# Splitting the gate weights earlier, and dividing the row sums one slot ahead, in a fused attention and mixture kernel

## The reference

```python
scores = scale * np.matmul(q, k.transpose(0, 1, 3, 2))
kth = np.partition(scores, -32, axis=-1)[..., -32:-31]
scores = np.where(scores >= kth, scores, -1e9)
attn = np.exp(scores - np.max(scores, axis=-1, keepdims=True))
attn = attn / (np.sum(attn, axis=-1, keepdims=True) + 1e-09)
x = (attn @ v), heads side by side           # 1152 x 512

rms = np.sqrt(np.mean(x * x, axis=-1, keepdims=True) + 1e-06)
xn = x / rms * rms_g
g = xn @ w_gate                              # 512 x 1536
x = (g * sigmoid(g) * (xn @ w_val)) @ w_out

expert_idx = np.argmax(x @ r_gate, axis=1)   # 8 experts, 288 places each
out[i] = gate_w[i] * relu(x[i] @ w1[e]) @ w2[e]
```

## Time and profile before

| | before |
|---|---|
| median of 3 runs | 669.05 us (667.72 to 669.4) |
| profiled execution | 668.76 us |
| its span | 667.0 us |
| PE busy | 615.8 us, 92% |
| DVE busy | 418.3 us, 63% |
| ACT busy | 326.3 us, 49% |
| POOL busy | 258.7 us, 39% |
| mean granted clock of PE | 0.984 of 2.4 GHz |
| chain that ended last | PE 76%, ACT 8%, POOL 6%, issue 4%, SP's queue 3% |

### The profile page before, as it was taken

The page is one execution under the profiler, slowest core; times in us unless marked ns, Lnnn a source line. Parts: engine busy times, 40 slices in busy tenths (PEclk is TensorE's granted clock), DMA queues, the critical chain, the costliest instruction groups (busy, mean ns, idle before and its releaser), DMA issues.

```text
span 667.0 us, 11082 instructions
## 1 busy us (share of the span) xinstructions
PE 615.8 (92%) x3914; PEld 475.3 (71%) x3914; DVE 418.3 (63%) x915; ACT 326.3 (49%) x713; POOL 258.7 (39%) x361
## 2 busy tenths in 40 slices
PE   5767879999999999999999999999989999999994
PEld 3445655775774775775765766756669999999994
DVE  4999899799699798898897997921111110111110
ACT  3485874765865766756756766742211011111110
POOL 1285874444544555464364463552310101111101
PEclk9997999999999999999999999999979999999998
DMA  9999200010010000000000000000395677667501
GB/s 187 339 373 371 59 18 1 1 33 0 1 33 2 12 22 1 18 17 0 17 17 2 1 17 0 1 17 0 130 391 186 216 230 276 223 223 283 167 1 37
DMA packets 53070, 65.45 MB, mean 98 GB/s; under 512 B 32218, under 2 KB 32218, under 8 KB 53020
## 3 DMA queue, kind: packets, MB, share of 16 engines
q1 hardware_dynamic: 51276, 60.05, 27.7%
q0 software_dynamic: 1744, 4.76, 2.0%
HBM read 52.89 MB, written 12.30 MB: 98 GB/s over the span
## 4 chain that ended last, share of the span: by engine, by line
PE 76%; ACT 8%; POOL 6%; issue 4%; SPq 3%; DMA 2%; DVE 1%; POOLq 0%; ACTq 0%
PE ps L746 11%; PE ps L760 11%; PE ps L514 11%; PE ps L501 8%; PE ps L505 7%; PE ps L502 7%; PE ps L482 5%; PE ps L455 4%; PE ps L466 4%; POOL s_ring L1409 3%; PE ps L440 3%; ACT pt L819 2%; DMA w_loads<-in_moe_w_gate 2%; POOL hid L1352 2%; ACT z_pair L957 1%
## 5 line engine op out<-in xcount | busy, mean ns | idle before, releaser
L1409 POOL TENSOR_TENSOR s_ring<-s_ring,z_pair 128x576 f32<-128x576 f32 x72 | 100.9, 1422 | 68.9 <-ACT z_pair L957 68.9
L1232 DVE MATCH_REPLACE8 w_top<-m,w_top 128x576 f32<-128x576 f32 x144 | 105.8, 742 | 0.0
L1228 DVE MAX8 m<-w_top 128x8 f32<-128x576 f32 x144 | 101.6, 746 | 0.0
L514 PE MATMUL ps<-wo_space,hid 128*128 128x512 f32 x216 | 99.3, 593 | 0.4 <-issue 0.4
L501 PE MATMUL ps<-w_parts,x_hi 128*128 128x512 f32 x216 | 90.2, 418 | 1.8 <-DVE w_parts L1161 1.1
L502 PE MATMUL ps<-w_parts,x_hi 128*128 128x512 f32 x216 | 85.4, 395 | 0.0
L746 PE MATMUL ps<-arena,w_loads 128*128 128x168 f32 x512 | 76.6, 312 | 0.6 <-ACT arena L819 0.6
L760 PE MATMUL ps<-arena,w_loads 128*128 128x168 f32 x512 | 75.9, 307 | 0.5 <-issue 0.5
L746 PEld LDWEIGHTS ps<-arena,w_loads 128*128 128x128 f32 x512 | 75.5, 195 | 1.0 <-ACT arena L819 1.0
L760 PEld LDWEIGHTS ps<-arena,w_loads 128*128 128x128 f32 x512 | 73.2, 190 | 0.6 <-issue 0.6
L1430 POOL DMA_INDIRECT out_rows<-arena,s_ring x16 | 15.1, 942 | 150.7 <-DVE arena L1256 113.6
(11 more groups left out here) (133 smaller groups left out, 875.3 us busy)
## 6 DMA issues: line engine op xcount, KB each, us to landing
w_loads<-in_moe_w SPq DMA_DIRECT2D x16, 2048.0 KB, 9.0
dispatched_rows<-drow SPq DMA_DIRECT2D x18, 260.0 KB, 7.2
w_loads<-in_moe_w_gate SPq DMA_DIRECT2D x1, 3072.0 KB, 11.7
w_loads<-in_moe_w_val SPq DMA_DIRECT2D x1, 3072.0 KB, 19.9
wo_space<-in_moe_w_out SPq DMA_DIRECT2D x1, 3072.0 KB, 14.1
arena<-dispatched_rows SPq DMA_DIRECT2D x8, 341.2 KB
out_rows<-drow SPq DMA_DIRECT2D x9, 256.0 KB, 5.3
q_space<-in_q SPq DMA_DIRECT2D x8, 256.0 KB, 3.0
```

The lines of the kernel that those rows point to most:

```text
L514: last = mm(blk[0], hid[:, c * P:(c + 1) * P], wo_s[:, c, :], start=(c == 0), stop=(c == CF - 1))
L1228: vec.max(m8[:, 2 * (n % 2) + a, i, :], w_top[:, a, :]).then_inc(s["top_step"], 1)
L1232: vec.match_replace(w_top[:, a, :], m8[:, 2 * (n % 2) + a, i, :], w_top[:, a, :], NEG).then_inc(s["top_step"], 1)
L1409: gp.tensor_tensor(row, row, z_pair[:, a, :], ALU.subtract).then_inc(s["lowered"], 1)
```

## The change

- SP issues `w_gate` right behind the first keys, and the keys of batch 1 ahead of the values of batch 0.
- The pieces are numbered anew: 0 to 5 are the gate's, 6 to 11 the value's. ACT writes their high parts in slots 0 to 3, 5 and 6 (two each, GAMMA); POOL writes all twelve low parts, in slots 1 to 7; `LOW_VECTOR` is gone. A block of tile 0 waits for the pieces that it needs, counted in the order of `LOW`.
- `divide(t, part)` takes the sum and the power out of `norm_first`. Part 0 (6 heads) runs on POOL at the end of slot 4t+3, in every tile, behind `dense(n, GAMMA)`; part 1 (2 heads) runs in slot 4t+4 behind the scaling.
- In group 3 alone ACT takes the second exponential ahead of the next scores' copies.
- For tile 0 alone, `low_part` runs on DVE inside the search of group 5, between its first replace pair and the next MAX8, instead of behind that search.
- For tile 0 alone, PE runs 2 extra matmuls (`bridge`) in slot 5.

```diff
-EARLY = (8, 3, 4, 3)
+EARLY = (8, 3, 4, 3, 2)
-HIGH = ((1, GAMMA), (1, GAMMA), (2, GAMMA), (2, GAMMA), (4, GAMMA), (5, BETA),
-        (5, GAMMA), (5, GAMMA), (6, ALPHA), (6, GAMMA), (6, GAMMA), (7, ALPHA))
-LOW = {0: (2, ALPHA), 1: (2, ALPHA), 2: (3, ALPHA), 3: (3, ALPHA), 4: (5, BETA), 5: (5, BETA), 6: (6, ALPHA), 7: (6, BETA), 11: (7, BETA)}
-LOW_VECTOR = {8: (6, GAMMA), 9: (7, ALPHA), 10: (7, ALPHA)}
+HIGH = ((0, GAMMA), (0, GAMMA), (1, GAMMA), (1, GAMMA), (2, GAMMA), (2, GAMMA),
+        (3, GAMMA), (3, GAMMA), (5, GAMMA), (5, GAMMA), (6, GAMMA), (6, GAMMA))
+LOW = {0: (1, ALPHA), 1: (1, ALPHA), 2: (2, ALPHA), 3: (2, ALPHA), 4: (3, ALPHA), 6: (4, ALPHA), 7: (5, ALPHA),
+       8: (6, ALPHA), 9: (6, BETA), 5: (6, GAMMA), 10: (7, ALPHA), 11: (7, BETA)}
+LOW_ORDER = tuple(LOW)
...
+            sp.dma_start(wg_raw, w_gate.rearrange("(c p) f -> p c f", p=P)).then_inc(s["wg_in"], 16)
+            key_rows(1, s["k_in1"])
             value_rows(0, s["v_in0"])
             q_tile(1, 0)
-            key_rows(1, s["k_in1"])
             sp.dma_start(gain[:], rms_g.rearrange("(c p) -> p c", p=P), allow_slow_non_contiguous=True).then_inc(s["g_in"], 16)
-            sp.dma_start(wg_raw, w_gate.rearrange("(c p) f -> p c f", p=P)).then_inc(s["wg_in"], 16)
             sp.dma_start(wv_raw, w_val.rearrange("(c p) f -> p c f", p=P)).then_inc(s["wv_in"], 16)
...
-                    pe.wait_ge(s["w_lo_set"], sum(p < m for p in LOW))
+                    pe.wait_ge(s["w_lo_set"], low_ready(i, bank is blk[1]))
...
+                if t == 0:
+                    pe.wait_ge(s["k1_copied"], KC)
+                    bridge(EARLY[4])
                 pe.wait_ge(s["normed"], 2 * t + 2)
...
                     if here:
                         probs(g, 0)
+                        if g == HP - 1:
+                            probs(g, 1)
...
-            def low_part(n):
+            def low_part(n, first=False):
                 t = due(n, ALPHA, XB)
-                if t is not None:
+                if t is not None and first == (t == 0):
...
                     if a == 0:
                         beside(n - 1, GAMMA)
+                low_part(n, True)
...
-            def norm_first(t):
-
-                pool.wait_ge(s["masked"], (t + 1) * H)
+            def divide(t, part):
+
+                h0, h1 = ((0, H - 2), (H - 2, H))[part]
+                pool.wait_ge(s["masked"], t * H + h1)
                 if t > 0:
                     pool.wait_ge(s["normed"], 2 * t)
-                gp.tensor_scalar(rden[:], den[:, t % 2, :], EPS_SUM, None, ALU.add).then_inc(s["den_step"], 1)
-                pool.wait_ge(s["den_step"], 2 * t + 1)
-                gp.tensor_tensor(rden[:], rden[:], nones[:], ALU.pow).then_inc(s["den_step"], 1)
-                pool.wait_ge(s["den_step"], 2 * t + 2)
+                gp.tensor_scalar(rden[:, h0:h1], den[:, t % 2, h0:h1], EPS_SUM, None, ALU.add).then_inc(s["den_step"], 1)
+                pool.wait_ge(s["den_step"], 4 * t + 2 * part + 1)
+                gp.tensor_tensor(rden[:, h0:h1], rden[:, h0:h1], nones[:, h0:h1], ALU.pow).then_inc(s["den_step"], 1)
+                pool.wait_ge(s["den_step"], 4 * t + 2 * part + 2)
+
+            def norm_first(t):
+
                 pool.wait_ge(s["t_free"], use["xa", t] + 1)
                 scale_rows(t, 0, H - 2)
+                divide(t, 1)
...
                 dense(n, GAMMA)
+                t = due(n + 1, GAMMA, XA)
+                if t is not None:
+                    divide(t, 0)
                 t = due(n, GAMMA, XA)
                 if t is not None:
                     norm_first(t)
```

More of the change, by code:

```diff
@@ L201, in build @@
             "disp_zero out_zero id_set z_set pchain v_padded "
-            "k_turned k_acted k_veced k1_copied w_hi_set w_lo_set w_low_veced "
+            "k_turned k_acted k_veced k1_copied w_hi_set w_lo_set "
             "t_full t_free vchain "
@@ L264, in split_piece, with low_ready @@
         def split_piece(m):
-            j = m // 2
-            raw, hi, lo = ((wg_raw, wg_hi, wg_lo), (wv_raw, wv_hi, wv_lo))[j % 2]
-            return raw, hi, lo, (2 * (m % 2), 2 * (m % 2) + 1), slice(j // 2 * 512, (j // 2 + 1) * 512)
+            raw, hi, lo = ((wg_raw, wg_hi, wg_lo), (wv_raw, wv_hi, wv_lo))[m // (2 * FB)]
+            j = m // 2 % FB
+            return raw, hi, lo, (2 * (m % 2), 2 * (m % 2) + 1), slice(j * 512, (j + 1) * 512)
         def pieces(table, n, at):
             return [m for m in (table if isinstance(table, dict) else range(len(table))) if table[m] == (n, at)]
+        def low_ready(i, gate):
+            first = 2 * i if gate else 2 * FB + 2 * i
+            return 1 + max(LOW_ORDER.index(first), LOW_ORDER.index(first + 1))
         def next_tile(n):
@@ L490, in ffn_block @@
                 if t == 0:
-                    m = 4 * i + (2 if bank is blk[1] else 4)
-                    pe.wait_ge(s["w_lo_set"], sum(p < m for p in LOW))
-                    if m > min(LOW_VECTOR):
-                        pe.wait_ge(s["w_low_veced"], sum(p < m for p in LOW_VECTOR))
+                    pe.wait_ge(s["w_lo_set"], low_ready(i, bank is blk[1]))
                 w_hi, w_lo = [w[:, :, i * 512:(i + 1) * 512] for w in parts]
@@ L529, in keep_running, with bridge @@
                     mm(tb[:, 0:384], ident[:], kT[0][:, 0, 0:384], start=True, stop=True)
+            def bridge(count):
+                for _ in range(count):
+                    mm(blk[1][:, 0:384], ident[:], kT[0][:, 0, 0:384], start=True, stop=True)
             def first_rows(c):
@@ L861, in split_weights @@
                     act.wait_ge(s["wg_in"], 16)
-                if m == 2:
+                if m == 2 * FB:
                     act.wait_ge(s["wv_in"], 16)
@@ L964, in probs @@
                 if t >= 2:
-                    act.wait_ge(s["den_step"], 2 * t - 2)
+                    act.wait_ge(s["den_step"], 4 * (t - 1))
                 row = s_ring[:, g % SR, a, :]
@@ L1040, in _ @@
                         score_rows(n + 1, 0)
-                    if here:
+                    if here and g != HP - 1:
                         probs(g, 1)
@@ L1155, in beside @@
             def beside(n, at):
[L1157 to L1162, removed]
                 for i in range(FB):
```

## The result

The changed kernel takes 695.07 us (median of 4 runs, 689.98 to 698.09) against 669.21 us before: ratio 1.038, 95% interval 1.0316 to 1.0444. The direction was forecast, the size was not: 679.7 us with a range of 674 to 685. The profiled execution took 692.41 us, its span 690.5 us against 667.0.

The account below looks back on a forecast made before the run. The prediction took DVE to bound the start and PE the tiles from about 120 us, with POOL's path at the seam deciding when PE goes on. 668.76 + 12.4 (seven divisions) - 1.5 (start) = 679.7 us, range 674 to 685.

Parts of the forecast that it names:

- PE already waits at the seam, so POOL's path counts in full: From slot 4t+3 to 4t+4, PE idles 0.15 us for POOL's path; all added time there lands on PE.
- 1.77 us a division: Six-head division on POOL at each seam: add 0.33, power about 1.36, next start 0.08 us; bounds 0.97 to 2.10.
- No slack elsewhere in the tile: PE idles only 1.17 us per tile, so nothing is given back: seven seams cost +12.4 us.
- The clock: PE's clock behind the new seam gaps of about 1.9 us: the forecast sum added nothing for it.
- The rival: PE's clock falls behind each of seven seams, 1.7 us each, 12 us more: about 692 us; 5% chance.
- The start, -1.5 us with its own division: Up to slot 8: -2.6 for the earlier last value block, -0.65 for POOL's multiply, +1.77 for the first division.
- The stalled search on the path: DVE stalls 2.6 us for x_hi inside the search begun at 59.81, delaying its end to 73.2 and POOL's next threshold.
- Low parts cost POOL 2.37 us each: In the start POOL gets three more low-part pieces, at 2.37 us each undisturbed.
- That VectorE is hardly faster at them: Low parts in the start: mean 2.49 us on POOL against 2.22 us on DVE, a ratio of 1.1.
- The 4.4 us a piece on POOL: By the skill's 1.96 ratio, three moved pieces lose the start some 6 us more, sum about 686; rejected for the trace.
- Range: Bounds 672 to 685.5 us from extremes of division and start, set to 674 to 685; forecast has 85%.

Follow-up runs that it names:

- small dose: Run 5: kernel before plus one unread one-column power on POOL at the eight seams; 672.63 us, ratio 1.0062.
- run 1: Changed kernel with the first division (6 heads) moved back to the front of norm_first in slot 4t+4; 668.65 us, ratio 1.000.
- run 8: Changed kernel with the division back in slot 4t+4 and ACT's high parts 8 and 9 in slot 4 instead of 5; 669.58 us, ratio 1.0019.
- run 9: run 6 plus 2 unread matmuls of 384 columns on PE in slot 5, filling its gap; 664.64 us, ratio 0.9946.
- run 10: run 9 plus ACT's high parts 8 and 9 in slot 4 instead of slot 5; 663.84 us, ratio 0.9944.
- run 7: Changed kernel with the division back in slot 4t+4 and tile 0's x_lo behind search 5 again; 670.55 us, ratio 1.0029.
- run 6: Changed kernel with the division back in slot 4t+4 and the last low part on DVE inside search 7; 664.45 us, ratio 0.9933.
- run 2: Kernel before with only the division ahead (6 heads at the end of slot 4t+3, 2 behind the scaling); 692.33 us, ratio 1.0327.
- run 3: Changed kernel with slot 4t+3's division one step earlier, ahead of the last value block's multiply; 670.16 us, ratio 1.0029.
- run 4: Changed kernel plus 2 unread matmuls of 384 columns on PE ahead of each seam's transposes; 684.04 us, ratio 1.0201.

## Why the prediction was right or wrong

- **PE already waits at the seam, so POOL's path counts in full: right.** The small dose shows it best: 0.54 us more gap for one small instruction.
- **1.77 us a division: right.** 1.80 us on POOL's timeline; the power of 6 columns took 1.37 us where the line between two rows gave 1.36. Periods without a drop take 49.9 us, as said.
- **No slack elsewhere in the tile: right.** Seven seams, 12.6 us against 12.4.
- **The clock: this step failed.** The sum put the clock behind the new gaps at nothing; it cost about 8.4 us of the profiled execution, 6.8 inside the seven periods and some 1.6 behind them. The rival had the right mechanism and the right price (1.7 us a seam), but for a drop at every seam, and 5% of the chance. I argued against it with a stretch in which PE was busy 13.40 of 16.91 us at full clock. That stretch has its idle time in gaps of 1.09 us and less; the change makes one gap of 2 us. A busy share over a long window says nothing on the single gap. The start had such gaps ahead of drops, of 1.57 us ahead of 49.52 us (the clock of 0.82 in the earlier trace rows is behind it) and of 2.06 us ahead of 59.89, and I took from there the price but not the warning. PE's timeline before, with 2.40 us for products that take 1.31 at full clock:

```profile
59.89 0.63 PE L466 MATMUL ps<-ident,s_ring 128*128 128x128 f32 x4 [2.06 <-ACT pt L819]
...
61.38 2.40 PE L482 MATMUL ps<-pt,arena 128*64 128x128 f32 x20 [0.42 <-ACT pt L819]
```

The Trainium skill (TensorE: Matmul & The Clock Gate, the HAM clock gate) says that the window in which the chip watches PE runs freely and is not reset when a kernel starts. By that rule equal gaps need not fare alike, and the traces agree: gaps of 1.95 us brought a drop at 416.13 and none at 314.42.

- **The start, -1.5 us with its own division, measured +2.55: wrong in three terms.** Together with the clock that makes up the miss: 4.1 + 8.4 of the 12.7 us between the 679.7 forecast and the 692.41 of the profiled execution. Without the division it was to be -3.3 and is about 0 by the medians of run 1. First, from the threshold behind search 5 to the subtraction I put 1.12 us, the row of a steady seam; it took 3.09, as ACT's marks stood behind both its copies and a copy that waited for PE at half clock (runs 8 to 10). Second, `x_hi` came at 66.1 instead of 65.2, and the threshold at 74.30 instead of 73.2. So the last low part ended at 98.41, not at 95.6 to 96.3. Third, the wait ahead of the last value block brought a drop there, about 1.5 us. I had one engine's list right, POOL's, and took the time of the lists that feed it from a place where they do not hold it up.
- **The stalled search on the path: wrong.** DVE stalled 3.43 us, which I priced at 2.6 us of delay. POOL's own list ended no earlier than the stalled search (74.22 and 74.17 us), and taking the stall away made nothing faster (run 7).
- **Low parts cost POOL 2.37 us each: right** (2.36 in the row above). **That VectorE is hardly faster at them: wrong.** The ratio of 1.1 came from a trace in which DVE's pieces ran beside POOL's work; run 6 has DVE at 1.22 us. The Trainium skill (GPSIMD Engine Reference, Performance versus the Vector engine) has a ratio of 1.96 for a two-input addition. The trace agrees, with 2.36 / 1.22 = 1.93. The 4.4 us a piece on POOL, which the prediction worked out with that ratio, scaled a time of DVE that POOL's work had drawn out. My ratio hid what run 6 then used, that a piece can be cheap on DVE.
- **Range.** Its upper end rested on extremes of the division's price and the start. Had the clock stood in it as an uncertain term of 0 to 8 drops at 1.7 us, it would have reached 699 us.

## What to carry to other kernels

Before an instruction is moved to an engine that is idle half of the time, look at what stands next to it in that engine's list: on one side of a waiting multiply the division cost next to nothing (0.3%), on the other the kernel lost 3.8%. Where the busiest engine waits, even briefly, for a path over other engines, every addition to that path counts in full, and an added gap of 2 us on PE must be priced twice, as the gap and as the clock behind it. When two engines end within a fraction of a microsecond of each other, removing one cause shows nothing; remove both before the cause is ruled out.

## What the runs showed of the hardware

**Short gaps of PE and its clock.** PE's gap ahead of the transposes of each seam, and whether a granted clock of 0.50 followed, in the traces of the kernel before, the changed kernel and runs 1 to 6:

| gap | seams | with a drop |
|---|---|---|
| up to 0.73 us | 41 | 0 |
| 1.22 to 1.31 us | 4 | 0 |
| 1.80 and 1.83 us | 2 | 0 |
| 1.87 to 1.99 us | 14 | 10 |
| 2.47 to 3.10 us | 3 | 3 |

A drop at a seam cost up to 1.7 us. Two matmuls of no use in the gap (0.40 to 0.50 us of it left at seven seams, 1.80 at the last) took all of them away. I had not expected gaps this short to do it. The table holds for seams, where PE is busy on both sides; in the start, where several waits stand close together, a gap of 1.57 us was followed by a drop too (kernel before, ahead of 49.52 us), and one of about 2.45 us, ahead of the last value block, was in the changed kernel and runs 1, 3, 4 and 7 but not in run 8.

**DVE and POOL side by side.** The subtraction of 128x1024 elements took DVE 1.22 us in run 6, and 1.85 to 2.60 us in the kernel before, where POOL was at work beside it. POOL's took 2.36 us in most places and 3.37 us where it began beside DVE's.
